# A two-layer MLP behind two attentions: first sums on GpSimd, a new order of head pairs, first slots spread anew, layer 2's first split moved

## The reference

```
q_d, k_d, v_d = mean over groups of 4 positions          # 144 positions
out_d = softmax(q_d k_d^T / 8) v_d, each row repeated 4 times
local = softmax over |i - j| < 4 of q k^T / 8, times v
x = (out_d repeated + local), heads side by side         # 2304 x 512
x = max(x @ w_in1, 0)**2 @ w_out1
y = softplus(x @ w_in2) @ w_out2,  softplus(h) = max(h, 0) + log1p(exp(-|h|))
```

## Time and profile before

| | us |
|---|---|
| median of 3 runs | 947.0 (941.35 to 950.98) |
| profiled execution, its own time | 948.02 |
| its span, first to last instruction | 946.1 |
| PE busy in the span | 902.5 (95%) |
| DVE, ACT, POOL busy | 606.3, 441.7, 321.4 |
| mean granted clock of PE | 0.978 |

### The profile page before, as it was taken

How to read it: one execution, slowest core, us unless ns; L and a number is a source line. 1 busy time by engine, 2 the same in 40 slices (tenths; PEclk the granted TensorE clock), 3 DMA queues, 4 the chain that set the end, 5 groups by cost and what they waited for, 6 DMA issues and landing times.

```text
span 946.1 us, 14913 instructions
## 1 busy us (share of the span) xinstructions
PE 902.5 (95%) x5767; PEld 841.2 (89%) x5767; DVE 606.3 (64%) x1069; ACT 441.7 (47%) x1077; POOL 321.4 (34%) x147
## 2 busy tenths in 40 slices
PE   7968779999999999999999799999999999999998
PEld 5768779999999999999989689899899998999997
DVE  2576756767667665655234477777776777777765
ACT  3557445463545545554456633533533534434433
POOL 2578967858596685857100000000000000000000
PEclk9979989999999999999999899999999999999999
DMA  9833204142312223100055310100200200100000
GB/s 246 294 139 130 80 1 143 68 130 80 131 59 89 76 68 105 43 26 1 2 170 155 112 37 1 43 26 1 67 1 1 68 1 1 67 1 1 34 1 34
DMA packets 24130, 64.56 MB, mean 68 GB/s; under 512 B 2454, under 2 KB 9622, under 8 KB 24060
## 3 DMA queue, kind: packets, MB, share of 16 engines
q1 hardware_dynamic: 24060, 63.62, 20.8%
HBM read 54.17 MB, written 9.44 MB: 67 GB/s over the span
## 4 chain that ended last, share of the span: by engine, by line
PE 83%; POOL 7%; DMA 3%; DVE 3%; issue 2%; ACT 1%; SPq 0%; POOLq 0%; ACTq 0%; DVEq 0%
PE bank L1172 21%; PE bank L1186 21%; PE bank L614 18%; PE bank L645 18%; POOL prod L373 3%; POOL w_lo L674 2%; POOL prod L419 2%; DMA vg<-in_v_grp 1%; DMA w_raw<-in_w 1%; PE bank L251 1%; PE bank L515 1%; PE bank L580 1%; PE bank L440 1%; PE bank L562 1%; DVE w_lo L674 1%
## 5 line engine op out<-in xcount | busy, mean ns | idle before, releaser
L614 PE MATMUL bank<-x_hi,w_hi 128*128 128x288 f32 x512 | 159.0, 311 | 14.0 <-DVE g_lo L634 6.5
L419 POOL TENSOR_TENSOR prod<-sc,vt 128x1344 f32<-128x1344 f32 x42 | 134.0, 3206 | 75.8 <-DVE sc L407 68.0
L614 PE MATMUL bank<-x_lo,w_hi 128*128 128x288 f32 x512 | 153.2, 299 | 0.0
L614 PE MATMUL bank<-x_hi,w_lo 128*128 128x288 f32 x512 | 153.1, 299 | 0.0
L645 PE MATMUL bank<-g_hi,w_hi 128*128 128x288 f32 x512 | 151.6, 296 | 0.0
L645 PE MATMUL bank<-g_hi,w_lo 128*128 128x288 f32 x512 | 151.5, 296 | 0.0
L645 PE MATMUL bank<-g_lo,w_hi 128*128 128x288 f32 x512 | 151.3, 296 | 0.0
L634 DVE TENSOR_TENSOR g_lo<-bank,g_hi 128x288 fp32r<-128x288 f32 x128 | 58.4, 456 | 142.2 <-ACT g_hi L629 142.1
L373 POOL TENSOR_TENSOR prod<-qt,kt 128x1344 f32<-128x1344 f32 x42 | 130.5, 3112 | 48.4 <-DVE sc L380 25.8
L926 ACT ACTIVATE sp_abs<-bank 128x384 f32<-128x384 f32 x96 | 47.1, 490 | 200.7 <-PE bank L1172 200.6
L1172 PE MATMUL bank<-x_hi,w_hi 128*128 128x384 f32 x384 | 130.6, 340 | 8.5 <-DVE x_lo L1081 6.4
(11 more groups left out here) (101 smaller groups left out, 1617.8 us busy)
## 6 DMA issues: line engine op xcount, KB each, us to landing
w_raw<-in_w SPq DMA_DIRECT2D x32, 512.0 KB, 5.0
kt<-in_k_loc SPq DMA_DIRECT2D x7, 960.0 KB, 4.9
vt<-in_v_loc SPq DMA_DIRECT2D x7, 960.0 KB, 4.7
kg<-in_k_grp SPq DMA_DIRECT2D x16, 288.0 KB, 3.8
qg<-in_q_grp SPq DMA_DIRECT2D x16, 288.0 KB, 3.1
vg<-in_v_grp SPq DMA_DIRECT2D x16, 288.0 KB
x_scratch<-ys SPq DMA_DIRECT2D x32, 144.0 KB, 3.4
x_raw<-x_scratch SPq DMA_DIRECT2D x6, 768.0 KB, 4.9
```

What stands on the lines that cost most here:

```text
L419: nc.gpsimd.tensor_tensor(dst, pb, win, ALU.mult).then_inc(prod_ready[m % 2], 1)
L614: last = nc.tensor.matmul(h_ps[f % 2][:, 0:NT], w[:, f, wc], x[:, T % 2, kc], start=(kc == 0 and i == 0), stop=(kc == KC - 1 and i == 2))
```

## The change

It does the following:
- q and k of a pair lie side by side in one array (`qk_first`, `qk`), loaded by one DMA, and one reduce sums both (`pool_qk`).
- The prologue's sums over four move from PE to POOL (`first_pool`, two adds per pair); the mask product uses rounded operands (`first_masks` on ACT makes them), one pass instead of more.
- The prologue's order of pairs is new on PE, ACT and DVE, and the order of SP's first loads; the mask of the local attention is made later on POOL.
- In slots 0 to 2 the steps of pairs, sums and additions are laid at other steps, `x_split_lo` comes earlier among POOL's products, and DVE takes six chunks of `weight_lo` in slot 0 instead of three. `LATE` is 9 instead of 10: seven loads of `w_raw` wait for the end of the prologue instead of six.
- `split_x2(0)` stands at the start of slot 7 on ACT and DVE instead of its end, and `W2_LAG` is 4 instead of 2.

```diff
-        LO_DVE = (9, 11, 13)
+        LO_DVE = (4, 6, 8, 10, 12, 14)
...
-        def first_sums(pe, j):
-            pe.wait_ge(first_qk[j], 32)
+        X0 = psum[5]
+
+        def first_pool(pool, j):
+            pool.wait_ge(first_qk[j], 16)
             if j:
-                pe.wait_ge(qk0_copied, j)
-            for s, src in enumerate((qg0, kg0)):
-                g4 = src[:, j].rearrange("p (g f) -> p g f", f=FACTOR)
-                for i in range(FACTOR):
-                    last = nc.tensor.matmul(QK0[:, s * G:s * G + G], ident[:], g4[:, :, i], start=(i == 0),
-                                            stop=(i == FACTOR - 1))
-            last.then_inc(qk0_summed, 1)
-
-        def first_sums_copy(a, j):
-            a.wait_ge(qk0_summed, j + 1)
-            nc.scalar.activation(qk0[:, j].rearrange("p s g -> p (s g)"), QK0[:, 0:2 * G],
-                                 ACT.Copy).then_inc(qk0_copied, 1)
+                pool.wait_ge(qk0_pooled, j)
+            two = qk_first[:, j].rearrange("p s (g f) -> p (s g) f", f=2)
+            half = pairs0[:].rearrange("p s g -> p (s g)")
+            nc.gpsimd.tensor_tensor(half, two[:, :, 0], two[:, :, 1], ALU.add).then_inc(pairs0_ready, 1)
+            pool.wait_ge(pairs0_ready, j + 1)
+            two = pairs0[:].rearrange("p s (g f) -> p (s g) f", f=2)
+            nc.gpsimd.tensor_tensor(qk0[:, j].rearrange("p s g -> p (s g)"), two[:, :, 0], two[:, :, 1],
+                                    ALU.add).then_inc(qk0_pooled, 1)
+
+        def first_masks(a):
+            a.wait_ge(ident_done, 2)
+            nc.scalar.activation(ident_r[0:BQ], ident[0:BQ, 0:BQ], ACT.Copy).then_inc(mask0_rounded, 1)
+            a.wait_ge(mask0_done, 2)
+            nc.scalar.activation(mask0_r[0:BQ], mask0[0:BQ], ACT.Copy).then_inc(mask0_rounded, 1)
...
-                last = nc.tensor.matmul(first_banks(j)[e][0:BQ, 0:NB * BK], ident[0:BQ, 0:BQ],
-                                        mask0[0:BQ].rearrange("p i k -> p (i k)"), start=False, stop=True)
+                last = nc.tensor.matmul(first_banks(j)[e][0:BQ, 0:NB * BK], ident_r[0:BQ],
+                                        mask0_r[0:BQ].rearrange("p i k -> p (i k)"), start=False, stop=True)
...
-        W2_LAG = 2
+        W2_LAG = 4
...
             first_load_v(0)
+            first_load(2)
+            first_load(3)
+            local_load_qk(1)
             first_load_v(1)
-            first_load(2)
-            local_load_qk(1)
             weight_load(sp, 0, w1)
-            first_load(3)
             first_load_v(2)
+            weight_load(sp, 1, w1)
             first_load_v(3)
-            for f in range(1, 5):
+            for f in range(2, 5):
...
+            for j in range(KC):
+                first_pool(pool, j)
+            score_mult(pool, 1, 0)
+            score_mult(pool, 1, 1)
+            pool.wait_ge(prod_ready[1], 1)
...
-            score_mult(pool, 1, 0)
-            score_mult(pool, 1, 1)
-            for i in range(2, NPROD):
-                lo(i - 2)
-                score_mult(pool, 1, i)
-            lo(4)
-            for i, f in enumerate((5, 6, 7, 8, 10, 12)):
-                lo(f)
-                value_mult(pool, 1, i)
-            lo(14)
+            lo(0)
+            lo(1)
+            score_mult(pool, 1, 2)
+            lo(2)
+            score_mult(pool, 1, 3)
+            lo(3)
+            score_mult(pool, 1, 4)
+            lo(5)
+            score_mult(pool, 1, 5)
+            lo(7)
+            lo(9)
+            value_mult(pool, 1, 0)
+            value_mult(pool, 1, 1)
+            lo(11)
+            value_mult(pool, 1, 2)
+            value_mult(pool, 1, 3)
+            lo(13)
+            value_mult(pool, 1, 4)
+            value_mult(pool, 1, 5)
             lo(15)
-            for i in range(NPROD):
-                score_mult(pool, 2, i)
-            x_split_lo(pool, 1)
-            for T in range(1, TILES - 1):
+            for T in range(TILES - 1):
+
+                x_at = min(2 * T + 2, NPROD) if T < 2 else 5 if T == 2 else NPROD
                 for i in range(NPROD):
-                    value_mult(pool, T + 1, i)
+                    if i == x_at:
+                        x_split_lo(pool, T + 1)
+                    if T + 2 < TILES:
+                        score_mult(pool, T + 2, i)
+                if x_at == NPROD:
+                    x_split_lo(pool, T + 1)
                 if T + 2 < TILES:
                     for i in range(NPROD):
-                        score_mult(pool, T + 2, i)
-                x_split_lo(pool, T + 1)
+                        value_mult(pool, T + 2, i)
...
-            first_sums_copy(a, 0)
+            first_masks(a)
             first_exp(a, 0)
             pair_exp(a, 0)
+            first_exp(a, 1)
+            pair_turn_copy(a, 0)
             for j in range(1, KC):
-                first_sums_copy(a, j)
-                pair_turn_copy(a, j - 1)
-                first_exp(a, j)
+                pair_exp(a, j)
+                if j + 1 < KC:
+                    first_exp(a, j + 1)
                 first_split_hi(a, j - 1)
-                pair_exp(a, j)
+                pair_turn_copy(a, j)
                 weight_hi(a, j - 1, 0)
-            pair_turn_copy(a, KC - 1)
-            weight_hi(a, KC - 1, 0)
             first_split_hi(a, KC - 1)
-            weight_hi(a, KC, 0)
+            weight_hi(a, 3, 0)
+            weight_hi(a, 4, 0)
...
+                if T == TILES - 1:
+                    split_x2(0)
...
-                    if local and f == (15 if T == 0 else 13):
+                    if local and f == (14 if T < 2 else 13):
...
+            first_norm(dve, 0)
+            first_max(dve, 1)
+            first_turn_copy(dve, 0)
             pool_v(dve, 0)
-            first_norm(dve, 0)
             pair_norm(dve, 0)
             for j in range(1, KC):
-                first_max(dve, j)
-                first_turn_copy(dve, j - 1)
                 first_norm(dve, j)
+                pair_max(dve, j)
+                first_turn_copy(dve, j)
+                if j + 1 < KC:
+                    first_max(dve, j + 1)
+                pool_v(dve, j)
                 first_split_lo(dve, j - 1)
                 pair_up(dve, j - 1)
-                pool_v(dve, j)
-                pair_max(dve, j)
-                for i in ((), (0,), (1, 2))[j - 1]:
-                    score_sum(dve, 1, i)
+                if j == 2:
+                    score_sum(dve, 1, 0)
                 pair_norm(dve, j)
-            first_turn_copy(dve, KC - 1)
-            score_sum(dve, 1, 3)
+            score_sum(dve, 1, 1)
             first_split_lo(dve, KC - 1)
             pair_up(dve, KC - 1)
-            pool_q(dve, KC)
-            pool_k(dve, KC)
-            score_sum(dve, 1, 4)
+            pool_qk(dve, KC)
+            pool_v(dve, KC)
+            score_sum(dve, 1, 2)
...
+                if T == TILES - 1:
+                    split_x2(0)
                 for s in range(FC):
                     hidden_lo(dve, T, s)
 
+                    if T == 0 and 1 <= s < 4:
+                        score_sum(dve, 1, s + 2)
...
-                    if T == 0 and s in (5, 7, 10):
-                        weight_lo(dve, LO_DVE[(5, 7, 10).index(s)], 0, w_lo_dve)
+                    if T == 0 and s in (0, 2, 5, 7, 9, 11):
+                        weight_lo(dve, LO_DVE[(0, 2, 5, 7, 9, 11).index(s)], 0, w_lo_dve)
...
+                            pair_max(dve, A)
                         if s == 1:
-                            pair_max(dve, A)
+                            pool_qk(dve, C)
+                            if T == 1:
+                                pool_v(dve, A)
                         if s == 2:
-                            pool_q(dve, C)
-                            pool_k(dve, C)
-                        if s == 3:
...
-            first_sums(pe, 0)
             first_scores(pe, 0)
             pair_scores(pe, 0)
-            for j in range(1, KC):
-                first_sums(pe, j)
-                first_scores(pe, j)
-                first_turn(pe, j - 1)
-                pair_turn(pe, j - 1)
-                first_x(pe, j - 1)
-                pair_scores(pe, j)
-            first_turn(pe, KC - 1)
-            pair_turn(pe, KC - 1)
-            first_x(pe, KC - 1)
+            first_scores(pe, 1)
+            for j in range(KC):
+                first_turn(pe, j)
+                pair_turn(pe, j)
+                if j + 1 < KC:
+                    pair_scores(pe, j + 1)
+                first_x(pe, j)
+                if j + 2 < KC:
+                    first_scores(pe, j + 2)
```

More of the change, by code:

```diff
@@ L912, in _ @@
                 output_copy(a, T)
-            def split_x2(i):
-                a.wait_ge(x2_loaded, 16 * (i + 1))
-                if i:
-                    a.wait_ge(h2_ready, FC * i)
-                for kc in range(KC):
-                    nc.scalar.activation(x2_hi[:, kc], x2_raw[:, kc], ACT.Copy).then_inc(x2h_ready, 1)
```

(41 more changed lines are left out.)

163 lines of the change are left out of this document (66 added, 97 removed).

## The result

| | before | after |
|---|---|---|
| median of 11 runs each | 944.8 (941.35 to 950.98) | 949.3 (947.52 to 952.10) |
| profiled execution, its own time | 948.02 | 948.48 |
| its span | 946.1 | 946.6 |

The change makes the kernel slower by 0.5%: ratio 1.005, 95% interval 1.0027 to 1.0073. The forecast was no change, 946 us. Yet the two profiled executions differ by 0.5 us only. A second profile of before (experiment 1) is therefore read beside the first.

The account below looks back on a forecast made before the run. PE's own work bounds settled two-pair slots. Prologue +7.4, slot 0 -5.3, slot 1 -2.6, slot 2 -0.8, slot 7 with layer 2 +0.4 sum to -0.9: 947.1, less 1.0 for the median, 946 us; range 932 to 958.

Parts of the forecast that it names:

- the last one of the sum: Whole kernel: 947.1 us for the profiled execution, less 1.0 because the runs' median lies 1.0 below it: 946.1.
- Prologue, +7.4: Prologue: the new loop over four engines, mostly at low clock, 15.2 us per pair, starts layer 1 at 67.7, +7.4 us.
- the 16.0 of the working: Prologue loop: summed durations per pair with PE at low clock, 16.0 us, against 11.8 at high clock.
- Slot 0, -5.3: Slot 0: the 5.11 us x_lo wait goes, a 4.7 us wait for pool_qk(5) comes; slot 65.4 us, -5.3.
- w_lo at about 2 us: Slot 0, sign to look for: each w_lo on DVE takes about 2 us; 1.95 beside POOL was assumed.
- rival C: Slot 0: DVE's six w_lo at 3.23 us each bound the slot, 957 us; decides from about 2.7 per w_lo; chance 0.16.
- Slot 1, -2.6: Slot 1: loses the low clock behind the 5.11 us wait, becomes 56.5 us, -2.6.
- Slot 2, -0.8: Slot 2: x_lo before the last two score products, becomes 56.4 us, -0.8.
- Slot 7, 64.2 us: Slot 7: the split's late load delays g_lo(7,0); PE idle 10.5 us plus 2.5 of low clock, 64.2 us, +1.3.
- Layer 2's first tile, 70.8: First tile of layer 2, 71.72 us before: starts at full clock, -1.6; two more weight splits, +0.7.
- A: Prologue: PE gets full clock, loop 11.8 us, -4.1 instead of +7.4, 935 us; chance 0.22.
- B: Slot 7: the split is hidden after all, -13 from 946, 933 us; chance 0.06.

Follow-up runs that it names:

- experiment 1: The kernel before, unchanged, run and profiled a second time: 942.9 us, ratio 0.998.
- experiment 7: Changed kernel with another order in the prologue's loop on DVE and ACT and v's group loads earlier: 937.8 us, ratio 0.9913.
- experiment 4: Changed kernel with matmuls that nobody reads added on PE in the prologue: 944.2 us, ratio 0.9998.
- experiment 5: Changed kernel with the load of pair 5's q and k ahead of the seven late w_raw loads: 946.2 us, ratio 1.0007.
- experiment 11: Changed kernel with the prologue of before, split_x2(0) at f=4 to 7, pair 5's load first, and W2_LAG back at 2: 926.9 us, ratio 0.9816.
- experiment 2: Changed kernel with the four copies of split_x2(0) at f=4 to 7 of slot 7 instead of its start: 938.4 us, ratio 0.9935.
- experiment 6: Changed kernel with three of slot 0's six w_lo (10, 12, 14) moved from DVE back to POOL: 956.2 us, ratio 1.0114.

## Why the prediction was wrong

**The step that failed is the last one of the sum**, "The median of the runs, 947.0, stands 1.0 below that execution". The stages' sum, -0.9, is a difference from one execution of before, and the step took that execution as typical but for 1.0 us, for before and after alike. It stood 3.2 us above the median of 11 runs of before (944.8, not 947.0), while after's profiled execution stands 0.8 below its own median. So of the 5.4 us between the forecast -0.9 and the +4.5 of the medians, 2.2 are the median of before, 1.8 the 1.0 taken off where 0.8 had to be put on, and 1.4 the terms below. What made that execution long was, as far as a second profile shows (experiment 1), low clock behind pauses where the other keeps the high one, or keeps it longer: 1.8 us in slot 7, 0.9 in layer 2, 1.1 in the prologue. The gains were sized by a long execution, the new costs by their own durations. Against the first profile the change is +0.5 us, against the second +4.7.

**Prologue, +7.4: right in mechanism, 1 us short.** Start 68.69 against 67.7. That pd of pair 1 ended at 34.2 as forecast is luck: pd of pair 0 ended at 18.25 instead of 19.0, and the loop took 15.94 us instead of 15.2. PE stayed low to the end of every stretch, so the 16.0 of the working would have been the value. The claim that nothing of the loop lies beside another part is borne out: another order made it 10.2 us (experiment 7). The Trainium skill, "TensorE: Matmul & The Clock Gate", Part 1, had it that throttled is the default; without the sums on PE it was, and filler lifted it for a part of the loops (experiment 4). POOL's sums took 1.15 and 0.67 us per pair and cost nothing, as forecast. (The sums that left PE are 8 matmuls a pair; 16 is the number of instructions that the trace shows for them.)

**Slot 0, -5.3: measured -3.9, with errors that cancel.** The wait for pair 5 was forecast at 4.7 and measured 5.18, with its cause shown by experiment 5; the 5.11 us for x_lo went. What the term left out is the rest of the chain over DVE and POOL: 1.52 us for pd behind a w_lo of 3.61, and 2.57 for xs behind POOL's value products. So the waits are 9.27 us, 4.6 more than forecast, while PE's busy time, 57.53 us, is 3.2 less than the 60.7 of the other terms (56.2 + 2.3 + 2.2): the low clock lasted shorter than taken (at the slot's start 3.5 us with matmuls of 0.44 us instead of 0.29, in before 5.2; behind the pause some 2.6 us), and the slot has 15 matmul records fewer than the settled one (428 against 443). "w_lo at about 2 us" is the mean of the six (13.2 us, 2.2 each), but two took 4.05 and 3.61. This is a weak form of rival C; its threshold of 2.7 us was not reached.

**Slot 1, -2.6: right but for 0.5 to 0.8 us** (-2.1 and -1.8). **Slot 2, -0.8: did not come** (+0.1). Its row said so: PE busy 56.99 of 57.18 us at clock 1.00, so the excess over the settled slot is PE's own work, and no wait was there to remove.

**Slot 7, 64.2 us: right** (64.05, pause 10.12 against 10.5; load and last x_lo came 2.2 to 2.4 us later than forecast, and so did the slot). **Layer 2's first tile, 70.8: too long**, 68.65. The +0.7 for two weight splits was wrong (experiment 11), and the tile of the earlier trace rows held a fall of the clock behind a pause of 2.13 us that the second profile of before and after's do not have (some 1.5 us).

**Rivals.** A (full clock in the prologue) did not occur by itself; made by filler for a part of the loops, it is worth 5.1 us (experiment 4), 6.3 at the start less what slot 0 takes back. For all loops it was never reached. B (the split hidden) did not occur; experiment 2 made it true by another place: -10.9 against the -13 given. C fell with experiment 6, but for its weak form above.

Not settled: what decides whether the clock falls behind a pause of about 2 us, and why the short loop, with PE idle 1.2 of 10.2 us, stayed low.

## What to carry to other kernels

Before subtracting costs read from one profile, compare its own time with the median, and ask of each cost at low clock whether it is there in every execution; take two profiles of the kernel before where half a per cent matters. Work that is taken off the bounding engine does not shorten a stage that a chain of waits sets: count the loop over all engines, and try the order of the loop before the place of its work. A copy that waits for a late load belongs behind the step at which the load has landed, and steps ahead of its first use: here at steps 4 to 7 of 16, not at either end. And where a forecast comes out, look whether its terms did: three times here errors cancelled.
